# First layer's units one to three one slot sooner, first-tile reciprocals two search steps later, slice highs in halves between the copies of p

## What is computed

```python
scores = scale * np.matmul(q, k.transpose(0, 1, 3, 2))      # 2 x 8 heads, 576 x 576, head_dim 64
kth = np.partition(scores, -32, axis=-1)[..., -32:-31]
scores = np.where(scores >= kth, scores, -1e9)
attn = softmax(scores)
x = (attn @ v)                                              # as 1152 x 512
x = (x @ w_a) * (x @ w_b) @ w_out                           # 512 -> 1536 -> 512
p = probs / (probs.sum(-1, keepdims=True) + 1e-9)
out = sum(p[:, e:e+1] * (np.maximum(x @ w1[e], 0) @ w2[e]) for e in range(4))
```

## Time and profile before

| what | value |
|---|---|
| median of 3 runs | 807.98 us (807.98 to 808.04) |
| the profiled execution: its own time / its span | 809.86 us / 808.0 us |
| mean granted clock of PE | 0.989 |
| busy: PE, DVE, ACT, POOL | 783.6, 570.7, 426.0, 355.0 us (97%, 71%, 53%, 44%) |
| busy in 100 to 150 us: PE, DVE | 49.10, 50.00 us |
| share of PE in the chain that ended last | 86% |

### The profile page before, as it was taken

One profiled execution on the slowest core, in us unless ns is written; L12 is line 12 of the kernel. 1 busy time (PEld: TensorE's weight loads), 2 busy tenths in 40 slices (PEclk: granted clock), 3 DMA queues, 4 the chain that ended last, 5 costly groups with the idle time before them and its releaser, 6 DMA issues.

```text
span 808.0 us, 14321 instructions
## 1 busy us (share of the span) xinstructions
PE 783.6 (97%) x5232; PEld 694.2 (86%) x5232; DVE 570.7 (71%) x1139; ACT 426.0 (53%) x845; POOL 355.0 (44%) x327
## 2 busy tenths in 40 slices
PE   7787999999999999999999999999999999999998
PEld 6676888888888888888899899999899999989997
DVE  7899999999999999998447853563455544363423
ACT  4677877677777777776564522442134422343210
POOL 5767875554444445555342312471036511464100
PEclk9898999999999999999999999999999999999999
DMA  9341567444555674444577001300132002210101
GB/s 317 111 148 49 197 225 282 140 166 171 171 170 170 196 248 170 169 152 165 184 260 232 1 27 57 101 27 1 32 100 79 1 2 77 77 55 1 53 0 66
DMA packets 53765, 97.94 MB, mean 121 GB/s; under 512 B 5696, under 2 KB 28992, under 8 KB 53696
## 3 DMA queue, kind: packets, MB, share of 16 engines
q1 hardware_dynamic: 53552, 96.96, 35.7%
q10 hardware_dynamic: 144, 0.07, 0.0%
HBM read 86.00 MB, written 11.01 MB: 120 GB/s over the span
## 4 chain that ended last, share of the span: by engine, by line
PE 86%; ACT 4%; DVE 3%; issue 3%; POOL 2%; DMA 2%; SPq 0%; ACTq 0%; POOLq 0%
PE ps L750 24%; PE ps L682 21%; PE ps L598 17%; PE ps L583 8%; PE ps L543 5%; PE ps L496 4%; PE ps L512 3%; PE ps L552 2%; POOL p_sb L1331 1%; ACT p_sb L809 1%; DMA w_raw<-moe_w_a_in 1%; PE ps L510 1%; DMA w_raw<-moe_w_b_in 1%; DVE m L1093 1%; ACT s_sb L795 1%
## 5 line engine op out<-in xcount | busy, mean ns | idle before, releaser
L1093 DVE MAX8 m<-work 128x8 f32<-128x576 f32 x216 | 152.4, 746 | 0.0
L682 PE MATMUL ps<-x_hi,w_hi 128*128 128x256 f32 (+1 forms) x448 | 132.7, 296 | 0.8 <-DVE u_sb L1209 0.4
L750 PE MATMUL ps<-w_hi,h_lo 128*128 128x512 f32 x288 | 112.5, 391 | 0.0
L750 PE MATMUL ps<-w_lo,h_hi 128*128 128x512 f32 x288 | 112.4, 390 | 0.0
L750 PE MATMUL ps<-w_hi,h_hi 128*128 128x512 f32 x288 | 112.3, 390 | 0.0
L1331 POOL TENSOR_TENSOR p_sb<-s_sb,p_sb 128x576 f32<-128x576 f32 x72 | 101.5, 1428 | 20.3 <-ACT p_sb L801 20.3
L1099 DVE MATCH_REPLACE8 work<-m,work 128x576 f32<-128x576 f32 x144 | 105.9, 742 | 0.0
L1414 POOL TENSOR_TENSOR u_sb<-u_sb,p_sb 128x256 f32<-128x256 f32 (+1 forms) x32 | 31.6, 988 | 161.0 <-DVE u_sb L1222 161.0
L1229 DVE TENSOR_TENSOR c_sb<-ps,p_sb 128x256 f32<-128x256 f32 (+1 forms) x32 | 14.7, 458 | 117.8 <-PE ps L682 117.8
L682 PEld LDWEIGHTS ps<-x_hi,w_hi 128*128 128x128 f32 x448 | 84.4, 188 | 2.5 <-DVE u_sb L1209 0.6
L938 ACT ACTIVATE h_hi<-c_sb 128x256 fp32r<-128x256 f32 (+1 forms) x32 | 14.2, 444 | 119.4 <-DVE c_sb L1229 119.4
(11 more groups left out here) (139 smaller groups left out, 2034.0 us busy)
## 6 DMA issues: line engine op xcount, KB each, us to landing
wo<-wo_d SPq DMA_DIRECT2D x96, 512.0 KB, 4.9
w_raw<-moe_w_in SPq DMA_DIRECT2D x32, 256.0 KB, 3.2
w_raw<-moe_w_in SPq DMA_DIRECT2D x16, 512.0 KB, 4.8
wo_d<-wo SPq DMA_DIRECT2D x12, 512.0 KB, 4.0
w_raw<-moe_w_a_in SPq DMA_DIRECT2D x4, 768.0 KB, 6.4
w_raw<-moe_w_b_in SPq DMA_DIRECT2D x4, 768.0 KB, 5.5
wo_raw<-moe_w_out_in SPq DMA_DIRECT2D x12, 256.0 KB, 6.1
x_d<-x_out_sb SPq DMA_DIRECT2D x9, 256.0 KB, 2.3
```

Of the source, the lines that this page charges most:

```text
L682: mm = nc.tensor.matmul(ps[:, bank, 0:NH[g]], w, x, start=first and c == n == 0, stop=last and c == HK - 1 and n == 2, skip_group_check=True)
L750: mm = nc.tensor.matmul(ps[:, DOWN_BANKS[j], 0:DM], h[:, f, tok], w[:, f, :], start=m == f == n == 0, stop=m == FM - 1 and f == 1 and n == 2)
L1093: nc.vector.max(m8[:, par, i, 8 * r:8 * r + 8], work[:, i, :]).then_inc(ve_top, 1)
```

## The change

- **Units.** `units_of(n)` gives slot 5 the units 0 and 1, slot 6 unit 2, slot 7 unit 3, slot 8 none, and from slot 9 on unit n-5 as before. So the second product of unit 1 moves from slot 6 to slot 5, the two of unit 2 from slot 7 to 6, the two of unit 3 from slot 8 to 7. ACT's copies move with them, and POOL's `product(u)` of units 0 to 3 (`product_of`). `h_transpose`, `h_out` and `send` stay in their slots; `h_transpose` waits for one more copy of b, as the bank that it writes is in use by the next unit (`copied`).
- **Order in slot 5.** PE: `partial(3)`, the second product of unit 1, then the transposes of p. ACT: the copies of unit 0 stand between the two exponentials, those of unit 1 after `p_out`. POOL: `product(0)` between the two halves of the last slice's low part.
- **Reciprocals** of the first tile after 12 search steps in all of the four searches (before 10, 10, 10, 8).
- **ACT in slots 1 to 4** is written out in `first_tile_slot`: `denominators` ahead of the scores of pair n+1; the slice's high part in two halves, one ahead of each head's `p_out`; the last slice is done in slot 4 (before in slot 5).
- **FILL** 40, 14, 8, 8 (before 30, 14, 7, 7).

```diff
-        WARM, FILL = 8, (0, 30, 14, 7, 7)
+        WARM, FILL = 8, (0, 40, 14, 8, 8)
...
+        def units_of(n):
+            if n < LAG_AB:
+                return ()
+            if n <= 2 * PR:
+                return ((0, 1), (2,), (3,), ())[n - LAG_AB]
+            return () if unit(n - LAG_AB) is None else (n - LAG_AB,)
+        def product_of(n):
+            if n <= 2 * PR + 1:
+                return n - LAG_AB if LAG_AB < n <= 2 * PR else None
+            return unit(n - LAG_AB - 1)
+        def copied(u):
+            return u + 2 if u < PR - 1 else u + 1
...
-                pe.wait_ge(ac_b, u + 1)
+                pe.wait_ge(ac_b, copied(u))
...
-                if m == 0:
+                if m == 1:
                     partial(DK - 1)
-                elif m > 1:
+                    pe.wait_ge(po_w, SLICES.index((1, m)) + 1)
+                    pe.wait_ge(ac_b, m)
+                    up(wb_hi, wb_lo, ps_b, m, pe_b)
+                elif m is not None:
+                    pe.wait_ge(ac_a, m)
                     up(wa_hi, wa_lo, ps_a, m, pe_a)
...
+            def first_tile_slot(n):
+                j, extra = n - 1, HIGH_IN[n]
+                below_top(j, 0)
+                below_top(j, 1)
+                if n == 1:
+                    slice_hi(3)
+                else:
+                    x_first(n - 2)
+                exponentials(j, 0)
+                exponentials(j, 1)
+                denominators(j)
+                scores_out(n + 1, 0)
+                diagonal(j, 0)
+                diagonal(j, 1)
+                scores_out(n + 1, 1)
+                slice_hi_half(extra, 0)
+                p_out(j, 0)
+                slice_hi_half(extra, 1)
+                p_out(j, 1)
...
+                if n == LAG_AB:
+                    b_out(0)
+                    a_out(0)
                 if j is not None:
                     exponentials(j, 1)
...
+                if n == LAG_AB:
+                    a_out(1)
+                if ms:
+                    b_out(ms[-1])
...
-            FIRST_SUMS, SUMS, SCALE, LOW = (10, 10, 10, 8), 1, 10, 11
+            FIRST_SUMS, SUMS, SCALE, LOW = 12, 1, 10, 11
...
                 if n == PR + 1:
-                    for half in range(2):
-                        last_slice_low(half)
+                    last_slice_low(0)
+                    product(0)
+                    last_slice_low(1)
```

More of the change, by code:

```diff
@@ L661, in _ @@
                     p_transpose(pair_of(n), scaled_tile(n + 1))
[L662 to L667, removed]
+                if m is not None and m > 1:
+                    if m < PR:
+                        pe.wait_ge(po_w, SLICES.index((1, m)) + 1 + m // (PR - 1))
+                    pe.wait_ge(ac_b, m)
+                    if u is not None:
+                        pe.wait_ge(ac_h, 2 * u + 2)
                     up(wb_hi, wb_lo, ps_b, m, pe_b)
@@ L831, in x_first, with p_out, a_out, b_out @@
                 copy(xu[:, cols], ps_x[:, cols], ACT.Copy).then_inc(ac_x0, 1)
[L833 to L839, removed]
+            def p_out(n, head):
+                act.wait_ge(pe_pT, 2 * n + head + 1)
+                act.wait_ge(pe_x, n)
+                chunks = KC - 1 + head
+                copy(pT[:, head, 0:chunks, :], ps_pT[head][:, 0:chunks * P].rearrange("p (c t) -> p c t", c=chunks),
+                     ACT.Copy).then_inc(ac_pT, 1)
+            def a_out(m):
+                act.wait_ge(pe_a, m + 1)
+                act.wait_ge(po_h, m)
+                copy(a_sb[:], (ps_y if m == 1 else ps_a)[:, 0:FS], ACT.Copy).then_inc(ac_a, 1)
+            def b_out(m):
+                act.wait_ge(pe_b, m + 1)
+                act.wait_ge(po_h, m)
+                copy(b_sb[:], ps_b[:, 0:FS], ACT.Copy).then_inc(ac_b, 1)
             def inv_turned(t):
@@ L973, in _ @@
             slice_hi(0)
-            for n in range(LAST + 1):
-                j, m, u = pair_of(n), unit_of(n), turned_unit(n)
+            scores_out(1, 0)
+            scores_out(1, 1)
+            slice_hi(1)
+            slice_hi(2)
+            def first_tile_slot(n):
[17 more added lines that the diff above has]
+                p_out(j, 1)
+            for n in range(1, LAG_AB):
+                first_tile_slot(n)
+            for n in range(LAG_AB, LAST + 1):
+                j, ms, u = pair_of(n), units_of(n), turned_unit(n)
                 for g in CHUNKS_IN.get(n, ())[0:2]:
@@ L1004, in _ @@
                     scores_out(n + 1, 1)
-                if j is not None and j < PR:
-                    diagonal(j, 0)
-                    diagonal(j, 1)
                 if u is not None:
                     h_out(u)
-                if m is not None:
-                    act.wait_ge(pe_a, m + 1)
-                    act.wait_ge(po_h, m)
-                    copy(a_sb[:], (ps_y if m == 1 else ps_a)[:, 0:FS], ACT.Copy).then_inc(ac_a, 1)
+                if ms and n > LAG_AB:
+                    a_out(ms[0])
                 if n == NP + 1:
@@ L1029, in _ @@
                     inv_turned(scaled_tile(n + 1))
-                for i in HIGH_IN.get(n, ()):
-                    slice_hi(i)
                 if finished_tile(n) is not None:
                     x2_out(finished_tile(n))
-                if m is not None:
-                    act.wait_ge(pe_b, m + 1)
-                    copy(b_sb[:], ps_b[:, 0:FS], ACT.Copy).then_inc(ac_b, 1)
+                if n == LAG_AB:
+                    a_out(1)
+                if ms:
+                    b_out(ms[-1])
                 if n == NP + 1:
@@ L1140, in between @@
                 t = scaled_tile(n)
-                if 1 <= n <= PR and done == FIRST_SUMS[n - 1]:
+                if 1 <= n <= PR and done == FIRST_SUMS:
                     first_sums(n - 1)
@@ L1374, in _ @@
                     limits(j)
-                if u is not None:
-                    product(u)
+                if product_of(n) is not None:
+                    product(product_of(n))
                 if j is not None:
```

38 lines of the change are left out of this document (14 added, 24 removed).

## The result

The changed kernel takes **812.87 us** (median of 5 runs, 812.45 to 814.64). The kernel before was at 807.98 beside it (5 runs, 807.36 to 809.90). The ratio is **1.0061, 95% interval [1.0045, 1.0078]**: slower by 4.9 us, where 806.3 was forecast. The profiled execution of the changed kernel has a span of 810.5 us and an own time of 812.45, that of before 808.0 and 809.86.

What follows compares the result with a forecast made beforehand. A loop of ACT and PE was taken to bound slots 5 to 8; PE's packed part behind slot 9 could only begin earlier. 2.1 us sooner less 0.4 for slot 8 gave 1.7 off the median 807.98: 806.3, range 804.0 to 808.3.

Steps and rivals of the forecast that it cites:

- Slot 6: ACT/PE loop in slot 6 takes 9.45 us where it took 11.74; masking of slot 7 at 81.9, 1.4 sooner.
- Slots 7 and 8: Slot 7 keeps 10.16 us; slot 8, without a unit, saves 0.7 on ACT; masking of slot 9 is 2.1 sooner.
- Slot 6, clock: PE at full clock from 77.7 on, held with little confidence; 1.4 us gained, or 0 if the clock falls.
- rival A: Half clock also in slot 6, so only slot 8's 0.7 less 0.4 is left: 807.6 us; chance 0.23.
- Slot 1, clock: PE's gap ahead of the diagonal products shrinks from 3.85 to 1.9 us, but the clock still falls at 26.5.
- rival B: The longer fill keeps PE's clock in slot 1; all is 1.9 us sooner, time 804.4; chance 0.25.
- Slots 2 to 4: Search 3 starts 1.5 us sooner; in slots 3 and 4 no reciprocal waits, last copy of p 0.4 sooner.
- Of 5.0 us of waits on DVE, 0.4 reach ACT's loop.: First tile: removing DVE's 5.0 us of waits makes the last copy of p only 0.4 us sooner, at 59.7.
- Slot 5: Gets more work: masking of slot 6 at +12.7 after the last copy of p, was +11.43; 0.8 us later.
- x_low: x_low of tile 1, awaited by PE before unit 4, ends 2.1 us sooner, moving with POOL's subtractions.
- The empty slot 8: PE gaps of 2.7 us within 3.6 may bring half clock; cost taken as 0.4 us, up to 1.7.
- rival D: Slower: empty slot 8 lowers the clock for two stretches and slot 6 is at half: 809.6 us; chance 0.09.

Runs made afterwards that it cites:

- two places: Changed kernel with a second place for h_sb, used by units 1 and 3, so POOL's product need not wait for the previous unit's transposes: 806.72 us, 0.9982.
- product behind: Changed kernel with POOL's product of units 1 to 3 put after both subtractions of p in its slot: 806.60 us, 0.9974 of the kernel before.
- the kernel before with zeros in slot 6: Kernel before with 8 zero matmuls added ahead of p's transposes in slot 6, nothing else changed: 808.25 us, 0.9987.
- the order alone: Changed kernel with units in old slots, FILL 30 in slot 1 and old reciprocal places, leaving ACT's order of slots 1 to 4: 805.63 us, 0.9954.
- the order with zeros in slot 6: Kernel with only ACT's order of slots 1 to 4, plus 8 zero matmuls ahead of p's transposes in slot 6: 805.07 us, 0.9964.
- late units: Changed kernel with all units, their copies and POOL's products back in their old slots, the rest kept: 805.29 us, 0.9962 of the kernel before.
- the kernel with late units and FILL 30: Changed kernel with all units back in their old slots and FILL 30 in slot 1 in place of 40: 805.49 us, 0.9964.

## Why the prediction was wrong

The step that failed is the one headed **"Slot 6"** ("is where it is earned"), with "Slots 7 and 8" built on it. Its loop, product 2.12, copy and chunks 1.42, 5.9 us from the masking copy to `h_out`, took the 5.9 from a slot 7 in which POOL's product was over before the subtraction could begin, and went past the wait inside `product` for the transposes of the unit before. POOL in the timeline of the kernel before, slot 7 (lines of that kernel):

```profile
82.50 1.01 POOL L1357 TENSOR_TENSOR h_sb<-a_sb,b_sb 128x384 f32<-128x384 f32 x1 [0.77 <-issue]
84.14 2.83 POOL L1331 TENSOR_TENSOR p_sb<-s_sb,p_sb 128x576 f32<-128x576 f32 x2 [0.63 <-ACT p_sb L801]
```

The product ends at 83.51, and the subtraction waits for ACT's masking copy alone. The wait was in the code, and the prediction moved the product a slot ahead without asking where its releaser stood. The changed kernel took 12.8, 11.6 and 12.7 us for slots 6 to 8; the two kernels without the wait took 9.8, 10.2 and 10.1 (two places) and 9.8, 10.2 and 10.4 (product behind), for 9.5, 10.2 and 10.1 forecast. The priced loop was right for a kernel in which this wait doesn't exist. That the repaired kernel's 806.6 lies beside the forecast of 806.3 is in part luck: its group had the kernel before at 808.53, so by its ratio it stands at 805.9 beside 807.98. Its trace is 2.5 us better than forecast from search 1 to mask 6 (53.4 against 72.4 - 16.45 = 55.95) and 0.9 worse from there to unit 4. Against these 1.6 us stand the 1.9 by which the profiled execution of before lay above the median.

- **Slot 6, clock.** Full clock was forecast from 77.7 on, with 0.23 for rival A. A happened: half clock from 75.98 to 79.39, at a cost of 1.3 us. Its premise, that gaps of PE are left in slot 6, held, but the largest, 2.03 us, was only 0.32 in the kernels without POOL's wait, which had no half clock there. By itself A was forecast at 807.6, not slower than before.
- **Slot 1, clock.** Forecast to fall again, with 0.25 for rival B. B happened: full clock from 26.5 to 33.3, and x_first of slot 2 at 30.57, before 32. Of the profiled executions of kernels with FILL 40, eight of eight had full clock there; of those with FILL 30 (or the kernel before), three of six. FILL 40 alone was worth 0.17%, 1.4 us, for the 1.9 of rival B. The rule set beside rival B (the Trainium skill, TensorE: Matmul & The Clock Gate, "Why this matters for your kernels": long gaps between bursts take the clock down) agrees in direction with that count, which is small. The gaps were 0.7 to 1.6 us with FILL 40 and 1.8 to 3.9 with FILL 30, and half of the executions with the longer ones kept their clock.
- **Slots 2 to 4.** "No wait is left": right, and from slot 1 on. Search 5 at 54.47 (57.6 forecast) has B's 1.9 in it and 0.8 from the earlier start of search 1.
- **"Of 5.0 us of waits on DVE, 0.4 reach ACT's loop."** That DVE's waits hardly count was right (1.0013 for the later reciprocals alone). That the slots gain only 0.4 was wrong: ACT's order takes 4.5 us off the distance from search 1 to mask 6 (50.6 against 55.1). Of these the half clock at 26.5 to 33.3 explains 2.5 to 2.9 (52.6 with FILL 40, and 52.2 in the kernel before with zeros in slot 6, whose profiled execution had full clock there), which leaves 1.6 to 2.0 for the order. Runs at the same granted clock don't settle it: at 0.994 the order alone had spans of 802.2 and 803.3, the kernel before a median of 804.8, but at 0.989 it had 802.9 (one run) against 807.8. The ratio says 3.7, with 2.7 at the near end of its interval; where all of the rest comes from was not located. One part shows in a pair of executions with half clock in slot 1: the kernel before took 55.1 us from search 1 to mask 6 and the order with zeros in slot 6 took 52.1, so there the order is worth 3.0. The halves of the slice in the gaps ahead of `p_out` were priced by adding up ACT's instructions between the diagonals and the last copy. What also went away was a slice copy of 0.84 ahead of the next slot's masking, of which only "0.6 sooner" in slot 2 was counted.
- **Slot 5.** +12.7 forecast, +12.73 measured. The comparison with +11.43 was the wrong one, though: with late units and ACT's new order it is 10.7, so the price of the early units in slot 5 is 2.0 and not 1.3.
- **x_low.** "POOL's end moves with the masking copy, 2.1 sooner, so I let x_low end 2.1 sooner": the tie was right. In the changed kernel POOL's second subtraction ends at 110.43 (109.00 + 1.43) and x_low at 110.97, 0.54 later, as in the earlier trace rows (107.94 and 108.48). In all twelve experiments it is 0.54 to 0.56 as well, though x_low takes 1.32 to 1.78 by the record. So x_low is done half a microsecond after POOL's subtraction, and unit 4 waits for it by 0.4 to 1.5 us in every experiment. In the changed kernel alone it doesn't, as PE, at half clock, comes later. The Trainium skill (SBUF — State Buffer, "Who interferes with whom") says that a DVE instruction with two SBUF inputs contends with a GpSimd one that reads SBUF, and the trace agrees.
- **The empty slot 8** was priced at 0.4, up to 1.7. In the changed kernel the half clock lasted for 10.2 us, and slot 6 was at half as well: both conditions of rival D came true, and D had the direction right, with a chance of 0.09. But D alone, at 809.6, doesn't reach the measured time. Taking the half clock of slot 8 away gave 1.3 us, taking the wait away, with the half clocks that went with it, gave 6.4 to 7.0.
- **The sum was made against an execution 1.9 us above the median.** The prediction said so and subtracted from the median. It didn't ask what the 1.9 was. The time of one and the same kernel goes with its granted clock, as 80 of the 83 runs of the kernel before beside the experiments show (the other three fit in):

| mean granted clock | runs | median span, us |
|---|---|---|
| 0.994 | 10 | 804.8 |
| 0.992 | 26 | 806.2 |
| 0.991 | 13 | 806.3 |
| 0.989 | 26 | 807.8 |
| 0.985 to 0.987 | 5 | 808.5 |

The profiled 808.0 was one of the 0.989 executions, with two stretches of half clock at 26.5 to 33.3. A gain "full clock in slot 1" is in part a gain that many executions of the old kernel have already: FILL 40 took 2.5 us off that distance in the trace and 1.4 off the median.

## What to carry to other kernels

When a step is moved a slot ahead, list every semaphore that it waits for and ask in which slot the releaser stands now: a buffer with one place ties the producer of unit u to the consumer of unit u-1, and in the same slot the producer is held up by all that stands ahead of the consumer on its engine, and holds up all that stands behind itself. Put such a step last in its slot, or give the buffer a second place; here either was worth 6 to 7 us. And test the parts of a change by themselves: one of four (ACT's order, itself several moves) made the whole gain, and one cost more than all of it.

## What the runs showed of the hardware

- **The same gap of PE is not always followed by half clock.** In the kernel with late units and FILL 30, PE stood for 3.54 us ahead of the products with the diagonals and the clock stayed at full; with the order alone and zeros in slot 6 it stood for 3.29 us there and ran at half from 25.1 to 31.9. PE in the timeline, the first of these kernels:

```profile
15.67 6.67 PE L612 MATMUL ps<-zero 128*128 128x128 f32 x51
25.87 2.05 PE L518 MATMUL ps<-diag,p_sb 128*128 128x128 f32 x16 [3.54 <-ACT diag L834]
```

and the second:

```profile
15.77 5.19 PE L612 MATMUL ps<-zero 128*128 128x128 f32 x45
24.25 3.05 PE L518 MATMUL ps<-diag,p_sb 128*128 128x128 f32 x16 [3.29 <-ACT diag L837]
```

Over the six executions with FILL 30 the gap and the half clock don't go together: 2.30, 3.29 and 3.85 us were followed by it, 1.78, 2.55 and 3.54 were not. Where two of the kernels have the same code up to slot 6, the longer gap was the one that fell (3.85 in the kernel before, 2.55 with zeros in slot 6; 3.29 in the order alone with zeros in slot 6, 1.78 without). So the length of the gap may change how often the clock falls, but didn't decide it in one execution. What decides it in one execution was not settled.
- **Executions of the kernel before spread by 3.7 us with their granted clock** (804.8 to 808.5 above), as much as the best versions gain. The four medians of the kernel before lie within 0.2% of each other; single executions don't.
- **The record of one instruction can be two lengths for one end.** x_low of tile 1 was recorded with 1.32 to 1.36 us in eight kernels and with 1.76 to 1.78 in six, and 0.69 for the next tile in all, yet it ended 0.54 to 0.56 us behind POOL's subtraction in all fourteen.
